# Routing a mixture of experts in two stages: the tokens of three of six chunks routed during attention, all tokens under the first expert tiles

## The reference

```python
for t in range(S):
    m_new = np.maximum(f_gate[:, :, t] + m, i_gate[:, :, t])
    f_stab = np.exp(f_gate[:, :, t] + m - m_new)
    i_stab = np.exp(i_gate[:, :, t] - m_new)
    C = f_stab[:, :, None, None] * C + i_stab[:, :, None, None] * np.einsum('bhd,bhe->bhde', vt, kt)
    n = f_stab[:, :, None] * n + i_stab[:, :, None] * kt
    y[:, :, t] = o * np.einsum('bhde,bhe->bhd', C, qt) / np.maximum(np.abs(nq), 1.0)
```

```python
for s in range(S):
    fresh_e = int(np.argmax(logits[b, s]))
    e = fresh_e if (s == 0 or local_gate[b, s] < 0.5) else prev_e
    prev_e = e
    h = np.maximum(x[b, s] @ w1[e], 0.0)
    out[b, s] = p[e] * (h @ w2[e])
```

## Time and profile before

| | us |
|---|---|
| median of 3 runs (lowest, highest) | 270.14 (269.42, 271.93) |
| the profiled execution, its time | 268.93 |
| the profiled execution, its span | 267.0 |
| busy: PE, DVE, ACT, POOL | 245.8, 176.9, 124.5, 70.2 |
| mean granted TensorE clock | 0.961 of full speed |

### The profile page before, as it was taken

The page is one execution under the profiler, slowest core; times in us unless marked ns, Lnnn a source line. Parts: engine busy times, 40 slices in busy tenths (PEclk is TensorE's granted clock), DMA queues, the critical chain, the costliest instruction groups (busy, mean ns, idle before and its releaser), DMA issues.

```text
span 267.0 us, 5876 instructions
## 1 busy us (share of the span) xinstructions
PE 245.8 (92%) x2097; PEld 185.5 (69%) x2098; DVE 176.9 (66%) x358; ACT 124.5 (47%) x187; POOL 70.2 (26%) x81
## 2 busy tenths in 40 slices
PE   5989997999999999676989999999999999999980
PEld 1677985889889898432469888888666666666550
DVE  6698989998989989678919889973313333322130
ACT  2236859679786884460015666552232332232310
POOL 7073308042260300010420332323222322320111
PEclk9999999999999999957599999999999999999997
DMA  6999578997998936958159882111010011100000
GB/s 151 283 211 321 134 265 256 247 395 182 334 284 305 290 51 200 366 182 258 30 143 356 316 284 94 31 34 34 31 39 29 10 34 33 34 26 24 7 26 21
DMA packets 14481, 42.37 MB, mean 159 GB/s; under 512 B 3827, under 2 KB 5933, under 8 KB 14458
## 3 DMA queue, kind: packets, MB, share of 16 engines
q1 hardware_dynamic: 12458, 37.54, 45.6%
q0 software_dynamic: 1824, 4.35, 5.5%
q10 hardware_dynamic: 176, 0.17, 0.3%
HBM read 38.50 MB, written 4.99 MB: 163 GB/s over the span
## 4 chain that ended last, share of the span: by engine, by line
PE 77%; DVE 8%; DMA 6%; issue 3%; ACT 3%; SPq 1%; POOL 0%; DVEq 0%; POOLq 0%; ACTq 0%
PE psU L1003 20%; PE psS L982 10%; PE psS L825 6%; PE psO L847 6%; PE psS L968 5%; PE psO L968 5%; DMA rows<-in_gates 4%; PE psA L753 3%; PE psO L990 3%; PE psU L836 3%; PE psS L758 3%; PE psM L803 2%; PE psM L950 2%; PE psU L900 2%; PE psA L816 1%
## 5 line engine op out<-in xcount | busy, mean ns | idle before, releaser
L1003 PE MATMUL psU<-W,hidT 128*128 128x320 f16 (+1 forms) x384 | 54.8, 299 | 0.4 <-DVE hidT L1463 0.4
L1003 PEld LDWEIGHTS psU<-W,hidT 128*128 128x128 f16 x384 | 37.5, 98 | 14.7 <-issue 0.9
L536 POOL DMA_INDIRECT out<-rows,outid x16 | 16.2, 1010 | 73.6 <-DVE rows L1470 73.6
L982 PE MATMUL psS<-W,xT 128*128 x128 | 28.9, 379 | 0.0
L847 PEld LDWEIGHTS psO<-W,hidT 128*128 128x128 f32 x192 | 25.2, 192 | 2.1
L1447 DVE TENSOR_TENSOR xT<-psM,xT 128x384 f16<-128x384 f32 x15 | 8.4, 558 | 26.1 <-ACT xT L689 26.1
L825 PE MATMUL psS<-W 104*128 104x256 f32 x96 | 24.3, 385 | 0.0
L491 POOL TENSOR_TENSOR W<-W 128x640 f32<-128x640 f32 x6 | 9.3, 1544 | 54.6 <-DMA W<-in_kvo 36.0
L847 PE MATMUL psO<-W,hidT 128*128 128x41 f32 x192 | 23.5, 271 | 0.0
L982 PEld LDWEIGHTS psS<-W,xT 128*128 128x128 f16 x128 | 12.5, 98 | 13.5 <-issue 0.2
L567 ACT ACTIVATE W<-stage 128x1024 f16<-128x1024 f32 (+1 forms) x14 | 16.0, 1146 | 9.1 <-DMA stage<-in_w 9.0
(11 more groups left out here) (196 smaller groups left out, 473.5 us busy)
## 6 DMA issues: line engine op xcount, KB each, us to landing
stage<-in_w SPq DMA_DIRECT2D x9, 640.0 KB, 4.6
stage<-in_w SPq DMA_DIRECT2D x11, 512.0 KB, 5.4
W<-in_kvo SPq DMA_DIRECT2D x5, 968.0 KB, 6.8
W<-in_w SPq DMA_DIRECT2D x8, 512.0 KB, 4.6
W<-in_w SPq DMA_DIRECT2D x6, 640.0 KB, 6.0
rows<-in_w SPq DMA_DIRECT2D x5, 512.0 KB, 4.8
W<-in_qk SPq DMA_DIRECT2D x6, 416.0 KB
x_rows<-rows SPq DMA_DIRECT2D x12, 192.0 KB, 6.3
```

What stands on the lines that cost most here:

```text
L536: pool.indirect_dma_start(out[:, :], bass.IndirectOffsetOnAxis(ap=outid[:], axis=0), ybuf, None, bounds_check=TOK - 1, oob_is_err=False).t ...
L982: last = mm(psS[:, half], x[:, k * P:(k + 1) * P], w, start=(n == 0), stop=(n == len(terms(t)) - 1))
L1003: last = mm(psU[:, 0:DM], h[:, k * P:(k + 1) * P], w, start=(k == 0 and n == 0), stop=(k == FC - 1 and n == 2))
```

## The change

Routing is done twice. In chunks 4 and 5 the six blocks of 128 tokens of chunks 0 to 2 are routed, for experts 0 to 3 alone (`early_choice`, `early_fill`, `early_codes`, `early_slots`, `early_sources` on DVE, 43 steps up to `early_gates`, with small products inside `own_part` on PE). Up to 128 of their tokens an expert are tiles 0 to 3. All tokens are routed during tiles 0 to 4 (`route_choice` to `route_finish`, 76 steps): what the first four tiles have not taken goes to further tiles, tiles 4 to 7 being the first ones of experts 4 to 7. There may now be 24 tiles in all and not 19 (`TILES`); by the counts above there are 4 + 4 + 8 = 16 again. A loop over single tiles runs to tile 12, and one over pairs of tiles from there.

The update of the state in the last chunk is left out, with two of the fill products behind it; no later chunk reads that state. The products that filled PE's time while routing ran are gone. x of the last chunk is made in two halves behind `tile_low(0)`, and its transposes and logits stand behind `first_up(0)`.

The gate of a token no longer travels with its row through DRAM: small products put it in place (18 for tiles 0 to 3, 36 for the rest), and a row has 384 words, not 385.

Fourteen of the 40 low halves go from DVE to POOL (`POOL_PIECES`); ACT first scales such a piece in its slot (`scale_for_pool`). The `result` of a tile goes from DVE to ACT, but for the last two tiles. POOL takes a row list for `write` from `srcid` itself, or copies it in the loop. The constants change with this, and rows of x and of the output are stored chunk by chunk.

The diff, cut to its core:

```diff
-TILES = NT + E - 1
+TILES = NT + E + 4
+DYN = TILES - E
+N1 = 6
+SINGLES = NT + 1
...
+POOL_PIECES = (3, 7, 11, 13, 14, 15, 18, 19, 23, 24, 28, 29, 34, 39)
...
-        late_slot = [n % 9 for n in range(OWN)] + [6, 7, 8, 0, 1]
-        spread = [EARLY_LOWS + (LATE - EARLY_LOWS) * t // SPREAD_STEPS for t in range(SPREAD_STEPS + 1)]
+        late_slot = [(2, 3, 4, 5, 0, 1, 6, 7, 8)[n % 9] for n in range(OWN)] + [6, 7, 8, 0, 1]
...
+        def lows_done(eng, n):
+            by_pool = sum(x < n for x in POOL_PIECES)
+            wait_if(eng, s_wl, n - by_pool)
+            wait_if(eng, s_wp, by_pool)
...
+                lows_done(sp, n - SLOTS + 1)
...
+                of = (staged(n) if e < LAST_E else late_staged(n - LAST_E * PIECES))[p]
+                pool.tensor_tensor(low(e, i), of, high(e, i)[p], ALU.subtract).then_inc(s_wp, 1)
...
+            for c in range(1, 4):
+                chunk(c)
+                split_low(A_CHUNK * c - 1)
+            chunk(4)
+            split_low(13)
+            split_low(14)
+            split_low(15)
...
-            for t in range(3):
+            gather(0)
+            pool.wait_ge(s_p, NQ * NC)
+            for t in range(1, LAST_E):
                 gather(t)
-            for t in range(E - 1):
-                gather(t + 3)
-                write(t)
+            split_low(18)
+            split_low(19)
+            write(0)
+            split_low(23)
+            rows_written(pool, NC)
+            pool.wait_ge(s_rv, R_SRC)
+            gather(4)
+            gather(5)
+            write(1)
+            split_low(24)
+            gather(6)
+            write(2)
+            split_low(28)
+            write(3)
+            gather(7)
+            split_low(29)
+            pool.wait_ge(s_rv, R_GATES + 1)
+            gather(8)
+            write(4)
+            split_low(34)
+            gather(9)
+            write(5)
+            split_low(39)
+            write(6)
...
+            def scale_for_pool(n, of):
+                if n in POOL_PIECES:
+                    nc.scalar.activation(of, of, ACT.Copy, scale=WSC).then_inc(s_wm, 1)
...
+                scale_for_pool(n, staged(n))
...
+            def result(t):
+                act.wait_ge(s_y, t + 1)
+                wait_if(act, s_out, 16 * t)
+                nc.scalar.activation(ybuf, psU[:, 0:DM], ACT.Copy, scale=ptile[:, bass.ds(t, 1)]).then_inc(s_yk, 1)
...
+            split_high(LAST_E * PIECES - 1)
+            act.wait_ge(s_rv1, R1_SUB)
+            nc.scalar.activation(r1["exl"], r1["sub"], ACT.Exp).then_inc(s_ra1, 1)
+            highs(20, 21)
+            for b in range(B):
+                x_evac(2 * (NC - 1) + b)
+            tile_high(1)
+            first_hidden_high(0)
+            for b in range(B):
+                keep_rows(NC - 1, b)
+            keep_gates(ptile[:, 0:LAST_E], at_gates1, s_gp1, 1)
+            highs(22)
+            tile_high(2)
+            act.wait_ge(s_rv, R_SUB)
+            nc.scalar.activation(rt["exl"], rt["sub"], ACT.Exp).then_inc(s_ra, 1)
+            highs(23)
+            first_hidden_high(1)
+            result(0)
+            highs(24)
+            tile_high(3)
+            highs(25, 26)
+            first_hidden_high(2)
+            result(1)
+            highs(27, 28, 29)
+            tile_high(4)
+            first_hidden_high(3)
+            result(2)
...
+            highs(34, 35)
+            first_hidden_high(5)
+            result(4)
+            highs(36, 37)
+            tile_high(7)
+            first_hidden_high(6)
+            result(5)
+            highs(38, 39)
+            tile_high(8)
+            first_hidden_high(7)
+            result(6)
...
+                    if c == NC - 2 and j == 2:
+                        early_keys()
+                    if c == NC - 2 and j == 3:
+                        early_codes()
+                    if c == NC - 1 and j == 0:
+                        early_ranks()
+                    if c == NC - 1 and j == 1:
+                        early_slots()
...
+                if c < NC - 1:
+                    pe.wait_ge(s_ks, c + 1)
+                    if c > 0:
...
-            idle(psS[:, 1], GAP["x"])
-            for b in range(B):
-                x_transposes(2 * (NC - 1) + b, b, NC - 1)
-            idle(psS[:, 1], GAP["lift"])
-            for b in range(B):
-                logits(2 * (NC - 1) + b)
-            idle(psS[:, 1], GAP["key"])
...
-            idle(psS[:, 1], GAP["gather"])
+            def last_logits():
+                for b in range(B):
+                    logits(2 * (NC - 1) + b)
             tile_transposes(0)
-            idle(psS[:, 1], GAP["split"])
             first_up(0)
-            for t in range(E):
+            for b in range(B):
+                x_transposes(2 * (NC - 1) + b, b, NC - 1)
+            tile_transposes(1)
+            last_logits()
+            early_gates()
+            first_up(1)
+            keys()
+            tile_transposes(2)
+            down(0, 0, between=codes)
+            first_up(2, 4, ranks)
+            tile_transposes(3)
+            down(1, 1)
+            def slots():
+                slot_ids(at_ids, named, R_HOT).then_inc(s_ids, 1)
+            first_up(3, 5, slots)
+            down(2, 2)
+            tile_transposes(4)
+            slot_ids(at_dyn, named_dyn, R_NAMED).then_inc(s_dyn, 1)
+            first_up(4, 4, slot_gate_products)
+            tile_transposes(5)
+            down(3, 3)
+            for t in range(LAST_E, E):
...
+                if c == NC - 1:
+                    early_slots()
                 combine(0)
+                if c == NC - 2:
+                    early_choice()
+                    make_scale(c - 1)
+                    split_low(piece)
+                    weigh(2)
+                    combine(1)
+                    scale_old(1)
+                    keep_logits(2 * (c - 1))
+                    weigh(3)
+                    early_fill()
+                    combine(2)
+                    decay_state()
+                    add_state()
+                    early_codes()
+                    combine(3)
+                    return
...
+            def last_x():
+                tile_low(0)
...
+                for b in range(B):
+                    at = slice(H * b, H * (b + 1))
+                    hn = obuf[:, at, 0:D]
+                    vv.tensor_tensor(hn, hn, rd[:, at, None].to_broadcast([P, H, D]), ALU.mult).then_inc(s_hn, 1)
+                    dve.wait_ge(s_hn, NC + b)
+                    vv.scalar_tensor_tensor(out=xw[:, b].rearrange("p (h d) -> p h d", d=D),
+                                            in0=th.rearrange("p (h d) -> p h d", h=BH)[:, at], scalar=1.0, in1=hn,
+                                            op0=ALU.add, op1=ALU.mult).then_inc(s_xb, 1)
+                dve.wait_ge(s_xb, B)
+                dve.sem_inc(s_x, 1)
...
+            early_gates()
             tile_low(1)
-            for n in range(EARLY_LOWS - 2, EARLY_LOWS):
-                late_low(n)
-            def first_step(t, late):
-                first_hidden_low(t)
-                for n in late[:1]:
-                    late_low(n)
-                tile_low(t + 2)
-                for n in late[1:]:
-                    late_low(n)
-                result(t)
+            for b in range(B):
+                keep_logits(2 * (NC - 1) + b)
+            route_choice()
+            first_hidden_low(0)
+            route_fill()
+            tile_low(2)
+            lows(20)
+            route_codes()
+            lows(21, 22)
+            first_hidden_low(1)
+            route_ranks()
+            tile_low(3)
+            route_slots()
+            first_hidden_low(2)
+            route_sources()
+            route_rest()
+            last_sources()
+            tile_low(4)
+            first_hidden_low(3)
+            lows(25)
+            route_finish()
+            lows(26)
+            tile_low(5)
+            lows(27)
```

809 lines of the change are left out of this document (523 added, 286 removed).

## The result

Over four runs each the changed kernel took 284.44 us in the median (283.69 to 285.68) and the kernel before 271.03 (269.42 to 272.00): a ratio of 1.0505, 95% interval 1.0433 to 1.0577. It is 5% slower; the forecast was 257.7 us. Some executions of every kernel run at a lower granted clock and take longer: the ratios with their intervals leave these out as far as enough others are left, the medians and ranges take all. The profiled execution took 283.69 us, span 281.9, and the mean granted clock was 0.931, where it had been 0.961.

A forecast was written before the change was run, and what follows sets the result against it. The kernel was taken as bound by PE, but for a 30.58 us gap. 268.93 - 29.1 (gap) - 1.5 (state, fill) + 10.0 (PE work) = 248.3; waits of 8.2 give 256.5 profiled, 257.7 median; range 249.5 to 265.

The forecast's parts named there:

- (f): POOL and DVE hold each other up at three places where PE hangs on DVE: 1.5 us, between nothing and 9.3.
- rival 2: The lock: each of the three hits of (f) costs a whole low half, +7.8, 265.5 us; chance 0.13.
- Added to PE, 10.0: PE's extra work: 64 products 3.57 us, 114 small ones 6.4, ten transposes and sums 1.1, last x 1.8; together +10.0.
- (a): Chunk 4: piece 12's low half comes later, ACT waits for piece 15's load, and PE waits 1.8 us.
- (b): Last x: ACT makes two high halves before moving the transposed x out, so the last logits wait 0.7 us.
- (c): Tile 3: DVE does `route_ranks` and `tile_low(3)` while PE has only `down(1)`: a wait of 1.3 us.
- (d): Tile 4: the last source products, `last_sources` and `tile_low(4)` come behind `route_rest`: a wait of 0.8 us.
- (e): Last piece, 39: its slot waits for POOL's low half of piece 34 behind `write(4)`: 2.1 us, bounds 0.9 and 3.7.
- A skipped pass, under 0.3: Loop: one more skipped pass takes under 0.3 us, costed at nothing.
- rival 1: No waits: the hand-written order meets every deadline, 249.5 us, up to 252; chance 0.20.
- Rival 3: Weight supply sets the pace: SP's slots come free too late, nothing is gained, 268 to 271 us; chance 0.04.
- Rival 4: Slower, by POOL's low half: 7.9 us each if time is all per element, 275 us; chance 0.03.

The follow-up runs named there:

- experiment 3: The changed kernel with each of POOL's 14 low halves made in four instructions of a quarter each: 284.15 us.
- the single-loop kernel: The changed kernel with one loop of single tiles on every engine in place of the loops of singles and pairs: 290.78 us, 1.0774 of before.
- the best kernel: The changed kernel with eight late low halves on DVE, POOL's six in quarters, routing steps ahead of low halves, pair loop under one condition: 267.71 us, 0.9926 of before.
- experiments 1 and 2: 1: changed kernel, POOL's low halves replaced by two clears each, 266.65 us. 2: eight idle POOL subtractions added to the best kernel, 281.43 us.

## Why the prediction was wrong

**The step that failed is (f).** It saw the mutual exclusion in the earlier trace rows, 0.3 us on one side and 1.15 on the other, and took it once, half caught: 1.5 us, with 9.3 as its bound and 265.5 in rival 2. Measured: eight halves added alone cost 13.7 us, and with the halves shortened to clears the kernel loses 17.8, of the 26.7 us by which the result lies above the forecast. Three things were wrong in it. It counted only steps with two inputs in SBUF; one-input TENSOR_SCALAR is held as well, and the routing is full of them. It looked at three places where PE hangs on DVE and at steps of the routing; but eleven of the fourteen halves held some DVE instruction, seven of the eight under the tiles, and only two of these seven instructions are routing steps, since DVE is busy for 69 of 88 us in the tiles and most steps of the routing take 0.17 to 0.3. And it said halves are short against a tile, where the question was whether they are short against DVE's slack: with the routing under the tiles there was none.

Point by point, the profiled span against the sum:
- *The gap goes, the state goes, 16 tiles stay*: right.
- *Added to PE, 10.0*: too high. 24 small products took 0.75 us and 36 took 1.16, 0.031 to 0.032 each with their ends and not 0.056: 114 are 3.6, not 6.4. The Trainium skill's TensorE: Matmul & The Clock Gate, section Back-to-back issue gap, gives a floor of about 25 ns from start to start; the trace agrees, with 25 ns for 24 products of 4 columns.
- *(a) 1.8 in chunk 4*: the stop is there, 1.13 us at 87.37, but it ends with DVE and not with ACT and a transfer, and its cause is the halves beside it: DVE came to it without idle time from 82.12 on, 1.79 us of which are the hold of 82.97. The stop is 0.50 with clears and under 0.3 with quarters (experiment 3). The first tile came at 114.46, not near 110. Ten microseconds at a granted 0.55 follow the stop, and I first took the one for the cause of the other. It isn't shown: the single-loop kernel had a stop of 1.20 there, the full clock from 80 to 112 us, and its first tile at 114.09.
- *(b) 0.7*: 4.96 (3.27 and 1.69), two held instructions. In the best kernel, without them, 2.68: so 2 us too small by itself.
- *(c) 1.3* and *(d) 0.8*: 3.08 and 5.52. Without holds the one is 0.85 and the other 4.4 (3.43 and 0.94). So (c) was right but for the exclusion. (d) forgot that tile 4's gather and its landing stand behind the routing.
- *Tiles 6 and 7, nothing*: 4.35; 3.63 in the best kernel, which no step had.
- *(e) 2.1*: 2.84, ended by POOL's low half as said. A half took 2.62, within 2.5 to 3.9.
- *A skipped pass, under 0.3*: a stop of 2.14 for four passes of pairs.
- *The granted clock* had no term of its own: full was expected. It was 0.55 for ten microseconds from 88.52 on and 0.90 under the tiles, where PE was busy for 67.05 us; with clears, at 0.95, it was 63.70.
- *Rivals*: rival 1, no waits, fell with the stops of 20.75 us. Rival 2 had the mechanism and half of its size, with 0.13. Rival 3 fell with experiments 1 and 2: clears with the same waits took 17.8 us away, and idle halves that supply nothing gave 13.7 back. Rival 4 named POOL, by a duration that didn't come.

Without POOL's halves under the tiles, with the routing first and the exit repaired, the kernel takes 267.71: still 10 above the forecast. The stops of 12.27 us in the tiles, against 6.4 forecast for (b) to (f), hold 6 of them, and the first tile at 112.2, not near 110, holds 2. The other 2 aren't traced; the granted clock, 0.93 under the tiles, is a part.

## What to carry to other kernels

Work that is given from DVE to GpSimd isn't free when DVE is on the path: beside a GpSimd instruction that reads SBUF, a DVE instruction with two SBUF inputs, or a TENSOR_SCALAR on numbers in SBUF, waits for its end, and DVE's list with it. Here giving DVE 9.8 us more work and taking 21 from GpSimd made the kernel faster (284.44 to 280.44 us). Before the move, ask of each GpSimd instruction whether a DVE instruction of the held kinds will come beside it. Here it did for seven of the eight under the tiles, and the price is the whole GpSimd instruction, once: behind the held instruction DVE goes on. The seven idle halves of 2.62 us held DVE for 1.5 to 3.2 us each. In a trace, look for DVE instructions that take several times the shortest of their form.

## What the runs showed of the hardware

- A GpSimd clear (write only) holds TENSOR_SCALAR (1.19 us in place of 0.17) and a one-input cast of 16 numbers (1.98 in place of 0.16), but neither two-input instructions nor TENSOR_REDUCE. A GpSimd subtraction with two SBUF inputs holds TENSOR_SCALAR and the two-input instructions.
- In all traces together I took the DVE instructions that began beside one such GpSimd operation and by their usual length would have ended at least 0.25 us before it. All 85 with two SBUF inputs and all 41 TENSOR_SCALARs on two or more numbers in SBUF took 0.3 to 2.4 us longer. None of the 114 with an input in PSUM did (0.02 at most), nor did 24 RECIPROCALs and 4 TENSOR_REDUCEs.
- GpSimd's 128x1280 f32 subtraction to f16 took 2.62 us, a quarter of it (128x320) 0.79, a clear 1.16; DVE makes such a half in 1.49, and one of 1024 in 1.22.
- Passes of a loop that are passed over cost PE no stop over 0.3 us (3 passes), 2.14 (4 passes of pairs) and 4.92 (8 passes). From the first and the last, 8 cost 4.6 to 4.9 more than 3: an estimate of 1 us each, with some 3 hidden, by which the 4 passes of pairs would show 1 us and not the 2.14 that they did.
- The trace of before has the full granted clock up to 110 us. Those of all other kernels have one to three stretches of lower clock there, by windows of 10 us: at 20 to 30 us (0.66 and 0.83), between 30 and 60 (0.64 to 0.85) or at 90 to 110 (0.52 to 0.96). Their places differ between kernels with the same work up to there. What decides them wasn't found.
